# Fused attention, routed experts and dense block: index columns read ahead by SP, ids copied per expert, results stored by ScalarE

## The reference

```python
# 1 attention: x (8, 8, 512, 64), state (8, 8, 32, 64), per batch and head
a  = softmax(x @ state.T / 8);   xread = a @ state      # tokens read the state
a2 = softmax(state @ x.T / 8);   sread = a2 @ x         # the state reads the tokens
x  = concat(xread, sread) as rows (4352, 512)
# 2 routed experts: E = 8, F = 1024, each row to the one expert with the largest logit
logits = (x / (|x| + 1e-6)) @ (emb / (|emb| + 1e-6)).T / tau
e = argmax(logits);  gate = softmax(logits)[e]
x[rows of e] = gate * (relu(x[rows of e] @ w1[e]) @ w2[e])
# 3 dense block, 2048 wide
h = relu(x @ w_in);  out = (s * h * h + b) @ w_out
```

## Time and profile before

| | |
|---|---|
| median of 3 runs | 1670.77 us (1667.96 to 1678.34) |
| the profiled execution | 1677.52 us, its span 1676.0 us |
| PE / PEld busy | 1426.6 us (85%) / 1161.6 us (69%) |
| DVE / ACT / POOL busy | 665.0 / 506.5 / 204.0 us |
| attention, to the last pick of an expert | about 0 to 174 us |
| expert stage | about 198 to 895 us |
| dense block | about 895 to 1676 us |

### The profile page before, as it was taken

How to read it: one execution, slowest core, us unless ns; L and a number is a source line. 1 busy time by engine, 2 the same in 40 slices (tenths; PEclk the granted TensorE clock), 3 DMA queues, 4 the chain that set the end, 5 groups by cost and what they waited for, 6 DMA issues and landing times.

```text
span 1676.0 us, 23063 instructions
## 1 busy us (share of the span) xinstructions
PE 1426.6 (85%) x6875; PEld 1161.6 (69%) x6876; DVE 665.0 (40%) x1645; ACT 506.5 (30%) x977; POOL 204.0 (12%) x265
## 2 busy tenths in 40 slices
PE   5787348878777888679777999999999999999996
PEld 4565236656656766567666888888888888888885
DVE  5776323335434334433437423223232323232322
ACT  4654112334324223432423322222222222222221
POOL 1223211111111111111115000001000000000100
PEclk9887568988978999889889999999999999999998
DMA  9552452364634435463361000101010101010000
GB/s 209 116 136 58 107 73 34 32 145 90 139 80 95 80 34 97 78 141 31 34 140 43 23 17 12 38 0 50 0 50 0 50 0 50 0 50 0 26 1 25
DMA packets 74722, 99.95 MB, mean 60 GB/s; under 512 B 46392, under 2 KB 46520, under 8 KB 73664
## 3 DMA queue, kind: packets, MB, share of 16 engines
q1 hardware_dynamic: 61888, 69.42, 16.0%
q0 software_dynamic: 12800, 30.09, 12.5%
HBM read 70.97 MB, written 28.53 MB: 59 GB/s over the span
## 4 chain that ended last, share of the span: by engine, by line
PE 56%; DMA 23%; issue 7%; ACT 5%; DVE 4%; POOLq 2%; ACTq 1%; POOL 1%; SPq 0%; DVEq 0%
PE bank_a L1327 22%; DMA xg<-x_tok,g_idx 17%; PE bank_n L1346 11%; PE bank_t L1346 10%; PE bank_a L1261 5%; DMA g_idx<-slot_tab 4%; PE bank_n L1286 2%; PE bank_t L1096 1%; DVE w_lo L953 1%; POOLq L334 1%; DMA x_tok<-st_rows 1%; ACT w_hi L616 1%; ACT w_hi L624 1%; POOLq L331 1%; PE bank_n L1248 1%
## 5 line engine op out<-in xcount | busy, mean ns | idle before, releaser
L1031 DVE TENSOR_TENSOR sq<-rel 128x512 f32<-128x512 f32 (+1 forms) x144 | 100.9, 700 | 478.8 <-ACT rel L703 478.8
L703 ACT ACTIVATE rel<-bank_a 128x512 f32<-128x512 f32 (+1 forms) x144 | 82.8, 575 | 550.1 <-PE bank_a L1327 550.0
L1327 PE MATMUL bank_a<-y_hi,w_in_hi 128*128 128x512 f32 (+1 forms) x576 | 217.7, 378 | 0.1
L1327 PE MATMUL bank_a<-y_hi,w_in_lo 128*128 128x512 f32 (+1 forms) x576 | 217.3, 377 | 0.0
L1327 PE MATMUL bank_a<-y_lo,w_in_hi 128*128 128x512 f32 (+1 forms) x576 | 217.3, 377 | 0.0
L1248 PE MATMUL bank_n<-ident,xg 128*128 128x128 f32 x156 | 35.5, 369 | 170.8 <-DMA xg<-x_tok,g_idx 170.7
L1248 PEld LDWEIGHTS bank_n<-ident,xg 128*128 128x128 f32 x156 | 23.0, 183 | 179.6 <-DMA xg<-x_tok,g_idx 179.6
L1261 PE MATMUL bank_a<-w_hi,xg_hi 128*128 128x512 f32 x304 | 119.1, 479 | 6.6 <-issue 4.2
L1327 PEld LDWEIGHTS bank_a<-y_hi,w_in_hi 128*128 128x128 f32 x576 | 108.3, 188 | 21.4 <-issue 0.8
L1327 PEld LDWEIGHTS bank_a<-y_lo,w_in_hi 128*128 128x128 f32 x576 | 108.3, 188 | 20.8 <-issue 0.2
L1327 PEld LDWEIGHTS bank_a<-y_hi,w_in_lo 128*128 128x128 f32 x576 | 108.3, 188 | 19.8
(11 more groups left out here) (200 smaller groups left out, 2380.9 us busy)
## 6 DMA issues: line engine op xcount, KB each, us to landing
w_raw<-in_moe_w SPq DMA_DIRECT2D x16, 2048.0 KB, 13.2
moe_tok<-yg POOLq DMA_DIRECT2D x38, 256.0 KB, 4.2
x_tok<-x_rows SPq DMA_DIRECT2D x8, 1088.0 KB, 5.3
x_m<-in_x SPq DMA_DIRECT2D x8, 1024.0 KB, 8.7
y_rows<-moe_tok SPq DMA_DIRECT2D x8, 1024.0 KB, 5.2
win_raw<-in_moe_w_in SPq DMA_DIRECT2D x8, 512.0 KB, 9.3
w_raw<-in_moe_w_out SPq DMA_DIRECT2D x1, 4096.0 KB, 19.1
slot_tab<-ids,pos POOLq DMA_INDIRECT x40, 6.8
```

The lines of the kernel that those rows point to most:

```text
L703: nc.scalar.activation(rel[:, k, 0:cols], ps_g[k][:, 0:cols], ACT.Relu).then_inc(rel_ready, 1)
L1031: nc.vector.tensor_tensor(sq[:, 0:cols], rel[:, k, 0:cols], rel[:, k, 0:cols], ALU.mult).then_inc(sq_ready, 1)
L1327: last = nc.tensor.matmul(ps_g[n % 2][:, 0:cols], w[:, wc], a[:, c, 0:cols], start=(c == 0 and w is w_in_hi and a is y_hi), stop=(c == DC ...
```

## The change

Five edits, the first four in the expert stage.

1. A tile `idx_all` (128 x 43) holds all index columns. SP loads column 0 as soon as the ids are scattered, columns 1 to 3 after `tab_ready`, and the other 39 after the first gather has landed, one DMA with one `value_load` each; then only follow `load_win(0)` and the rest. POOL copies one column to `g_idx` with a tensor copy.
2. `moe_id` is no longer written tile by tile. SP copies the whole range of each expert (4352 ids) from `slot_tab` to `moe_id`, 8 DMAs, each after the one before has landed, behind `load_win(0)` and ahead of the load of w1 of expert 1.
3. ACT issues the store of `yg`; in its order the exponential and the square move ahead of `result`, and its wait for `gate_ready` ahead of the square goes.
4. DVE reads the logits of the gathered rows (`gate_logits`) ahead of `hidden_lo` instead of at the start of `gate_scale`.
5. The 8 splits of expert 0 on ACT and on DVE move from the batches of attention to its end; on DVE behind `tile_tab`.

```diff
@@ sync
-            sp.wait_ge(tab_ready, 1)
-            sp.wait_ge(st_stored, 16 * B)
+            def load_idx(g, done):
+                src = slot_tab[0:P, :] if g == 0 else slot_tab[ds(slots_of(sp, g), P), :]
+                sp.dma_start(idx_all[:, g:g + 1], src).then_inc(done, 16)
+            sp.wait_ge(slots_written, 16 * (TPB + 1) * B)
+            with nc.allow_non_contiguous_dma(reason="one word per row"):
+                load_idx(0, idx_first)
+                sp.wait_ge(tab_ready, 1)
+                for g in range(1, NEAR):
+                    load_idx(g, idx_next)
+                sp.wait_ge(gathered, 16)
+                for g in range(NEAR, NSLOT):
+                    load_idx(g, idx_loaded)
             load_win(0)
+            for e in range(E):
+                if e:
+                    sp.wait_ge(id_copied, 16 * e)
+                first_row = sp.value_load(tile_tab[0:1, 4 * NSLOT + 1 + e:4 * NSLOT + 2 + e], min_val=0, max_val=NTOK)
+                sp.dma_start(moe_id[ds(first_row, CAP), :].rearrange("(q n) o -> q (n o)", q=P),
+                             slot_tab[e * CAP:(e + 1) * CAP, :].rearrange("(q n) o -> q (n o)", q=P)).then_inc(id_copied, 16)
             for e in range(1, E):
                 sp.wait_ge(w1_ready, WS * e)
@@ gpsimd
-            def tile_ids(g, first):
...
-            def next_tile(g):
...
-            def store(g):
...
+            def gather(g):
+                if not starts(g):
+                    pool.wait_ge(gathered, 16 * g)
+                nc.gpsimd.tensor_copy(g_idx[:], idx_all[:, ds(g, 1)]).then_inc(idx_turn, 1)
+                pool.wait_ge(idx_turn, g + 1)
+                if not starts(g):
+                    pool.wait_ge(xg_tr, g)
+                    pool.wait_ge(gate_sq, g)
+                    pool.wait_ge(gate_lg, g)
+                    pool.sem_inc(gather_turn, 1)
                 nc.gpsimd.indirect_dma_start(out=xg[:], out_offset=None, in_=x_tok[:, :],
                                              in_offset=bass.IndirectOffsetOnAxis(ap=g_idx[:], axis=0)).then_inc(gathered, 16)
...
+            gather(0)
+            pool.wait_ge(idx_next, 16 * (NEAR - 1))
+            gather(1)
+            gather(2)
             last = last_tile(pool)
+            gather(3)
+            pool.wait_ge(idx_loaded, 16 * (NSLOT - NEAR))
             with pool.Fori(1, last) as g:
-                next_tile(g + 3)
-                store(g)
-            store(last)
+                gather(g + 3)
@@ scalar, in the loop over batches
-                split_hi(i)
@@ scalar, behind it
+            for k in range(2 * WS):
+                split_hi(k)
+            def store(g):
+                act.wait_ge(yg_ready, g + 1)
+                act.dma_start(moe_tok[ds(rows_of(act, g), P), :], yg[:]).then_inc(moe_stored, 16)
@@ scalar, tile(g)
                 next_w1(g + 1)
+                gate_soft(g + 2)
+                gate_square(g + 3)
                 result(g)
-                gate_soft(g + 2)
-                act.wait_ge(gate_ready, g + 3)
-                gate_square(g + 3)
+                store(g)
                 hidden_hi(g + 1)
@@ vector, in the loop over batches
-                split_lo(i)
@@ vector, behind tile_tab
+            for k in range(2 * WS):
+                split_lo(k)
@@ vector, tile(g)
                 gate_final(g + 2)
+                gate_logits(g + 3)
                 hidden_lo(g + 1)
```

More of the change, by code:

```diff
@@ L80, in attention_moe_ffn @@
         xg = sb(top, "xg", [P, RW], f32)
-        tile_tab = sb(top, "tile_tab", [P, 4 * NSLOT + 1], i32)
+        tile_tab = sb(top, "tile_tab", [P, 4 * NSLOT + 1 + E], i32)
+        idx_all = sb(top, "idx_all", [P, NSLOT], i32)
         gate_s = sb(top, "gate_s", [P, NSLOT], f32)
@@ L91, in attention_moe_ffn @@
         gi = sb(top, "gi", [P, 2], i32)
-        used = sum(-(-n // 32) * 32 for n in (4 * P, 4 * P, 2 * P, 2 * P, 4 * PAIRS * E, 4 * RW, 4 * (4 * NSLOT + 1), 4 * NSLOT,
+        used = sum(-(-n // 32) * 32 for n in (4 * P, 4 * P, 2 * P, 2 * P, 4 * PAIRS * E, 4 * RW, 4 * (4 * NSLOT + 1 + E), 4 * NSLOT, 4 * NSLOT,
                                               4, 4, 4, 4 * TROWS, 4 * E, 4 * E, 4 * E, 32, 8))
-        sb(top, "line_pad", [P, (-(-used // 128) * 128 - used) // 4], f32)
+        sb(top, "line_pad", [P, (128 - used % 128) // 4], f32)
         wts = ExitStack()
@@ L268, in attention_moe_ffn @@
         idx_loaded = sem("idx_loaded")
-        id_stored = sem("id_stored")
+        idx_first = sem("idx_first")
+        idx_next = sem("idx_next")
+        idx_turn = sem("idx_turn")
+        gather_turn = sem("gather_turn")
+        id_copied = sem("id_copied")
         gathered = sem("gathered")
@@ L309, in attention_moe_ffn @@
         GATE_STEPS = 16
+        NEAR = 4
         O_C = TROWS - HEAD
@@ L399, in _ @@
             sp.wait_ge(moe_stored, 16 * (HEAD + E + 2))
-            sp.wait_ge(id_stored, 16 * (HEAD + E + 2))
+            sp.wait_ge(id_copied, 16 * E)
             load_y(0, HEAD)
@@ L405, in _ @@
             sp.wait_ge(moe_stored, 16 * last + 16)
-            sp.wait_ge(id_stored, 16 * last + 16)
             sp.sem_inc(load_turn, 1)
@@ L456, in _ @@
                                                  in_=ids[0:n, bb, t:t + 1], in_offset=None).then_inc(slots_written, 16)
-            def tile_ids(g, first):
-                if not first:
+            def gather(g):
+                if not starts(g):
                     pool.wait_ge(gathered, 16 * g)
[L461 to L464, removed]
@@ L499, in _ @@
-            store(0)
+            gather(3)
+            pool.wait_ge(idx_loaded, 16 * (NSLOT - NEAR))
             with pool.Fori(1, last) as g:
-                next_tile(g + 3)
-                store(g)
-            store(last)
+                gather(g + 3)
+            pool.wait_ge(xg_ready, last + 2)
             pool.wait_ge(wout_loaded, 16)
@@ L713, in _ @@
             result(last)
+            store(last)
             for n in range(FC2):
@@ L960, in hidden_lo, with gate_logits @@
                     nc.vector.tensor_tensor(hid_lo[:, c], ps_ht[m][:], hid_hi[:, c], ALU.subtract).then_inc(hid_t_ready, 1)
+            def gate_logits(g):
+                dve.wait_ge(gathered, 16 * g + 16)
+                nc.vector.tensor_reduce(lg[:], xg[:].rearrange("p (q w) -> p w q", q=PAIRS)[:, P:P + E, :], X_AXIS, ALU.add)\
+                    .then_inc(gate_lg, 1)
             def gate_scale(g):
@@ L987, in gate_final @@
                 nc.vector.reciprocal(gate_s[:, ds(g, 1)], gc[:, 7:8]).then_inc(gate_ready, 1)
+            gate_logits(0)
             x_lo(0)
@@ L992, in _ @@
             gate_final(0)
+            gate_logits(1)
             gate_scale(1)
@@ L996, in _ @@
             gate_final(1)
+            gate_logits(2)
             gate_scale(2)
```

19 lines of the change are left out of this document (4 added, 15 removed).

## The result

The changed kernel takes 1511.99 us, the median of 4 runs (1511.19 to 1513.42), against 1673.39 us before in the same session (4 runs, 1667.96 to 1678.34): a ratio of 0.9037, with a 95% interval of 0.9005 to 0.9069. The forecast was 1510. The profiled execution has a span of 1510.9 us, 165.1 less than before.

A forecast was written before the change was run, and what follows sets the result against it. PE, waiting for late gathers and partly at lower clock, bounds the expert stage. 259.6 + 36 x 12.6 + 10.5 = 723.7 us, 160.7 less; execution 1516.8, less 6.7 of profiled excess, gives 1510 us, range 1470 to 1580.

The forecast's parts named there:

- The bound and the tile: Expert stage: PE waits for gathers, 179.6 us in 36 waits; without them a tile takes 12.6 us instead of 17.6.
- The old median of 10.1 fits already: Expert tiles: about 11 us are left for a gather to land, so even the old 10.1 us landing fits.
- Attention, 6 us off: End of attention: moving ACT's splits out of its chain saves 6 us, bounds 0 and 8.
- The start of the stage: Expert stage start: SP's 39 index loads delay the w_in slice; first ReLU 19 us later, tile 0 at 259.6 us.
- ACT's store: Expert tiles: register load, arithmetic and DMA issue, about 1.2 us ahead of `hid_hi`, hidden with some 3 us of cover left.
- the term of expert changes: At 7 expert changes, splits of new weights cost 1.5 us each, 10.5 in all, bounds 0 and 26.
- The copies: SP's 8 id copies ahead of expert 1's w1 load take 29 us, with nothing lost.
- slow gather: Rival, expert tiles: landings stay slow at 13.1 us, a tile takes 14.6, 72 us more, 1582 us; chance 0.08.
- slow copies: Rival, SP: id copies take 12 us each, w1 of expert 1 comes 40 us late, 1550 us; chance 0.05.
- slow index loads: Rival, stage start: SP's 39 loads do not overlap and cost 236 us instead of 45, 1701 us; chance 0.02.
- late ACT: Rival, expert tiles: store and square push `hid_hi` behind the end of `up`, 1 us a tile, 1546 us; chance 0.08.
- The faster start: Rival: index loads at the lower bound (-20), free expert changes (-10), attention 8 (-2), 1478 us; chance 0.17.

The follow-up runs named there:

- writes_back: Changed kernel with ids written tile by tile from POOL's queue ahead of each gather, without the 8 copies; 1603.05 us, ratio 0.9331.
- writes_behind: Changed kernel with ids written tile by tile from POOL's queue, right behind each gather instead of ahead; 1523.32 us, ratio 0.9081.
- after_again: Changed kernel unaltered, rerun on the same chip as others of its group; 1511.09 us, ratio 0.9048.
- splits_back5: Changed kernel with the splits of expert 0 back inside attention (fifth edit undone), more rounds; 1510.49 us, ratio 0.9028.
- early_win: Changed kernel with the first w_in slice ahead of all index loads, columns in three groups, id copies behind expert 1's loads; 1471.39 us, ratio 0.8807.
- win_first: Changed kernel with the first w_in slice loaded ahead of the 39 index loads instead of behind them; 1474.17 us, ratio 0.8582.
- writes_act: Changed kernel with ids written tile by tile from ACT's queue behind the store, without the copies; 1556.98 us, ratio 0.9319.
- ids_alone: Kernel before with only the second edit: SP copies ids per expert, no id write in POOL's loop; 1525.62 us, ratio 0.8894.
- after: The changed kernel itself, with all five edits, against the kernel before; 1511.99 us, ratio 0.9037.
- store_pool: Changed kernel with the third edit undone, the result store back on POOL's queue; 1505.83 us, ratio 0.8982.
- splits_back: Changed kernel with the splits of expert 0 back inside attention, earlier run on the slower chip; 1511.2 us, ratio 0.8797.
- after_third: Changed kernel unaltered, run once more on another chip to compare the store's place; 1515.51 us, ratio 0.9029.

## Why the prediction was right

**The bound and the tile: right.** The result of tile 36 was forecast for 723.7 us and came at 719.27. PE's waits for the gather went from 179.6 to 23.7 us, the granted clock to 0.98. A tile takes 12.22 us; I took 12.6. The issue of 0.64 us ahead of `up` is gone altogether, and the transposes take 0.87 instead of 1.02. This made the 36 tiles 13.7 us shorter than forecast.

**"The old median of 10.1 fits already": wrong, and without harm.** The wait is for gather, turn and three readers together, and writes_back shows 14.7 us a tile with such a gather. The other half of that paragraph, that the landing falls to 4 to 8 us once the write ahead of it is gone, was the one that carried: 3.5 us. It came from one row, the first gather, with its write behind it, and writes_behind shows that this reading was the right one.

**Attention, 6 us off: wrong.** The pick came 1.7 us later. Rows of a chain gave a price for the splits, but not what is late next; the store of `st_rows` was, with 14.39 us instead of 8.44. I had bounded the term by 0 and 8, and its value is 0 within the noise of the medians (after_again and splits_back5 differ by 0.6 us).

**The start of the stage: right in kind and size.** Forecast: the last index load at 234, first ReLU at 240.9, tile 0 at 259.6. Measured: the slice issued at 238.45, the first ReLU at 243.84, tile 0 at 263.78. The first index load went out at 188.44, 6.1 us late, for attention; with POOL's first copy (1.71 us beside the splits of DVE, 0.18 without them) the first gather landed 7.0 late. The loads gave 2.6 back, at 1.06 us each on most (0.27 for the register, 0.15 for its arithmetic, 0.33 for the issue, gaps between) instead of 1.15, the slice 1.3 (3.73 us instead of 5) and the copy and square behind it 0.2; 1.3 was lost again between ReLU and tile 0. The Trainium skill's floor of about 600 ns for a `tensor_load` ("DMA: Bandwidth & Descriptors", section "Latency and other measured facts") does not hold here: 39 of them take 0.27 us each. (By that page a load would come to 1.16 us, an estimate, and the 39 to 0.4 us more than the 1.15 each that I took; the 4 us of the forecast are against the 1.07 of the rows.)

**ACT's store: under-priced.** I put 1.2 us ahead of `hid_hi` and called it covered. Within an expert that holds. At 7 changes it costs 1.45 us each (the changes took 1.8 us each, forecast 1.5), and the first store 2.8: it sat 5.82 us in its issue, right behind SP's issues of w1, w_in and w2 of expert 1 (4.5 MB, 260.49 to 261.65). In early_win, where these loads go out behind it (from 233.35, the store at 224.83), it took 2.23, later ones 0.35. That the loads cause it is a reading of the traces; no run changed them alone. Together some 13 us of a change that was forecast to be free; the term of expert changes (10.5, bounds 0 and 26) had room for it.

**The copies:** 22.9 us for 8 (238.92 to 261.84), where 29 was forecast; hidden, as said.

So the forecast met the time within 2 us by some luck: a tile that was 0.4 us too long and the other terms cancelled. -13.7 for the tiles, +2.8 for the first store, +2.3 for the changes and +4.2 at the start give -4.4, which is what tile 36 shows. The rest is luck of another kind: I took off 6.7 us because the profiled execution of before was that much above its median, and that of after was only 0.6 above, which turns -4.4 into +2. Two sums of the forecast are a little off as well: its own bounds added up reach from 1470 to 1566, not 1475 to 1560, and its chances, with the 0.02 for a case in between, add up to 1.02. Of the rivals the slow gather, slow copies and slow index loads are out; late ACT came true at expert changes only. The faster start did not happen by itself, but win_first and early_win show that its 20 us and more were to be had. The Trainium skill's rule that each DMA engine serves the queues of both kinds in turn ("DMA: Bandwidth & Descriptors", section "SWDGE vs HWDGE vs iDMA") spoke for a slow gather behind ACT's store; the landings, 3.5 us with the store on either queue, show no such cost for rows of 2 KB, while writes_act shows one for single words.

By edits, in all columns but the first, and added in this order: the second alone brings 153 us (ids_alone). The first and fourth on top of it bring 27 (58 in tile 0 to 37, most of it at expert changes, less 27 for the start and 4 at the end: store_pool against ids_alone, in which the copies also stand at another place). The third loses 13 (after against store_pool). That is 167, of which attention took 2 back. The fifth is worth nothing. In another order the shares are others, as the gains overlap. On the chip where the kernel before takes 1716.8 us, the second alone takes off 191, the other four without it 114 (writes_back), and all but the fifth, which is worth nothing, 206 (splits_back); put on last, the second brings 92. The first and the fourth were not tried by themselves.

## What to carry to other kernels

Ask of every small DMA what stands behind it: 128 words written ahead of a gather cost 2.1 us a tile (14.7 against 12.6 on the mean of 37) even with its indices read ahead, the same words behind it 0.3 (12.9). Price a wait by what the last engine of the chain loses: POOL's 26.8 us in win_first cost PE 10. When register-addressed loads are gathered on one queue, put the one large transfer that an engine waits for ahead of them. An engine with much slack on average (ACT, 34% busy) can still be the late one at the places where extra work is stacked, and an issue moved to it should be priced there.

## What was not expected of the hardware

- A write of 128 separate words to HBM lands after 7.8 us in the median, ahead of the gather (before, 7.0 at least, 12.8 at most) or behind it (writes_behind, 6.5 and 13.4); 17 KB in 16 pieces land in 2.0 us.
- With such a write ahead of it on its queue, a gather of 128 rows takes 10.8 us on the mean from its issue to POOL's next copy (writes_back); with the write on another queue 8.6 (writes_act); without it 4.3 (after_again).
- The kernel before takes 1671.5 us on one chip and 1716.8 on another, and the code of splits_back 1510.5 and 1511.2 on the same two. The small writes, which only the first has, are the likely cause; they were not measured by themselves on both.
- The first store issue on ACT took 5.82 us where large loads had been issued on SP just before, though the queues are different ones (4.89 and 5.00 in after_again and after_third), and 2.2 to 2.5 in the five kernels in which none had been issued in the 24 us before it.
- A copy of 128 words on POOL takes 0.18 us, but up to 2.01 (the first in writes_behind) when it starts while DVE subtracts in a split of weights: it then ends with that instruction of DVE or the next.
